# A recurrent attention and two feed-forward layers on one core: the state's decay and part of the values' products moved to ScalarE, with another order of the queues

## The chip, the core and the metric

The kernel runs on one core of one Trainium2 chip. The metric is the device time of one execution in microseconds. TensorE is called PE here, VectorE DVE, ScalarE ACT, GpSimd POOL and SyncE, which issues the transfers, SP.

## The reference

Inputs are r, k, v of 4 sequences, 8 heads, 768 tokens and 48 channels, a decay w and a bonus u for each head and channel, and the weights of two layers. All is float32.

```
for t in range(S):
    cur = einsum('bhd,bhe->bhde', u * k_t, v_t)
    y[t] = einsum('bhd,bhde->bhe', r_t, state + cur)
    state = w * state + einsum('bhd,bhe->bhde', k_t, v_t)
h = relu(y @ w_in)                       # 384 -> 1024
a = conv over 3 tokens of h, by channel
x = (h * sigmoid(a)) @ w_out             # 1024 -> 384
out = x + relu(norm(x) * g @ w_ch1) @ w_ch2   # 384 -> 1536 -> 384
```

## The kernel before, in words

**Attention by chunks.** The 3072 tokens are cut into 24 chunks of 128 (CHUNKS, six to a sequence). Within a chunk the recurrence is a masked product. Chunk m goes through these steps, each a function of the kernel:

- `scale` (DVE, L710): r and k, channels first, times powers of w made at the start.
- `scores` (PE, L407): 16 products k by r into two PSUM banks. `masked` (DVE, L718) twice: the scores times a triangular mask, into `att`.
- `ruk` (POOL, L879 and L881): r*k*u by token. `dots` (DVE, L751): its sum over each head's channels, 8 numbers per token, in `c8`. `cv` (POOL, L894): v times these dots, the token's own term.
- `kd` (POOL, L888): k by token times a table of powers (`powkt`). `kv` (PE, L421): 16 products of it with v, the chunk's contribution to the state.
- `state` (DVE, L736, or L738 and L743): the old state plus that contribution (L738, twice), and then the whole times w to the 128th (L743). The first chunk of a sequence has one multiplication only (L736).
- `y` (PE, L442 and L447): r by the state, plus scores by v. `x_sum` (DVE, L758) adds the term of `cv`. `xt` (PE, L454): three transposes. `xh` (ACT, L556) and `x_low` (DVE, L765) write the high and the low part of the result into the columns that the layers read.

**Layers by units.** The two layers work on 7 units of 440 columns (UNITS). Each float32 product is split in three float32r products of high and low parts (`split_product`, L393 to L395). `mm1` 0 to 7 and `mm2` 0 to 7 are the first layer, `ffn1` 0 to 11 and `ffn2` 0 to 11 the second; each `mm1` or `ffn1` is 9 products. `relu`, `sig` and `hi` are ACT's work on a tile of the first layer, `conv`, `gated` and `low` are DVE's. `x2_hi`, `x2` and `x2_low` take over the first layer's result; `fhi` and `flow` make the second layer's tiles. `sums`, `total`, `square`, `variance`, `root` and `newton` make the norm.

**Order of work.** Each engine's queue is written out by hand: a list for everything up to the end of unit 0 (PE_FIRST, ACT_FIRST, DVE_FIRST, POOL_FIRST, SP_FIRST), and a list that is repeated for units 1 to 6 (PE_PLAN and so on). `each_unit` (L158) runs them. An entry such as ("y", 2) in a PLAN is the third chunk that belongs to the unit: the chunks of unit 0 are 4 to 6 (0 to 3 come ahead of it), of unit 1 they are 7 to 10, then 11 to 13, 14 to 17, 18 to 20 and 21 to 23; unit 6 has none. Steps in LATER are made for the next chunk, and steps in OF_STATE are left out for the last chunk of a sequence. `root` uses a square root, `sig` a sigmoid, and ACT loads a table (ACT_TABLE_LOAD) at each change between them; `table` (L594) is a one-column sigmoid that brings the load forward.

**The start.** DVE makes the powers of w (L668 to L687, a chain of some 30 small instructions that starts when w has been loaded). PE transposes the table (L548), DVE copies it to `powkt` (L840), and then chunks 0 to 3 run in banks that the layers don't use yet. The first product of the layers is ("mm1", 0) of unit 0, at L393. It needs the low part of the first piece of weights (`w_low`, L704). ("means", j) (L541) are six entries of the second layer's preparation each. SP issues every load, in the order of SP_FIRST.

In PE's lists the small float32 products (`scores`, `kv`, `y`, `xt`) stand between the layers' float32r products; a run of such neighbouring entries is called a stretch below.

## Time and profile before

| | |
|---|---|
| median of 3 runs | 633.79 us (632.58 to 634.89) |
| the profiled execution | 634.28 us |
| its span | 632.0 us |
| PE busy | 614.2 us, 97% of the span |
| DVE, ACT, POOL busy | 425.1, 259.0, 141.6 us |
| granted clock over the span | 1.00 |

The span runs from the first to the last instruction of the profiled execution; the 2.28 us between it and the execution's own time lie around it. Busy times are sums over the instructions of an engine, and a matmul's duration includes the time in which its successor has started, so durations on PE overlap; the distance from start to start is the rate.

### The profile page before, as it was taken

The numbers are of one execution on the slowest core, as the hardware profiler recorded it, in microseconds if no ns is written. First come the engines' busy times: TensorE is split into PE (matmuls) and PEld (weight loads), VectorE is DVE, ScalarE is ACT, GpSimd is POOL, SyncE is SP. The second block draws the span as 40 slices with busy tenths as digits, with TensorE's granted clock in tenths as the row PEclk, the third lists the DMA queues.
The fourth block names the chain that finished last, engine by engine and source line by source line (L and its number), as shares of the span: only waits on it lengthen the run. The fifth ranks groups of instructions, "written<-read, shape, count | busy, mean of one in ns | idle before, by whom it ended". The sixth has DMA issues, their size and how long they took to land.

```text
span 632.0 us, 10918 instructions
## 1 busy us (share of the span) xinstructions
PE 614.2 (97%) x4434; PEld 561.2 (89%) x4434; DVE 425.1 (67%) x689; ACT 259.0 (41%) x466; POOL 141.6 (22%) x139
## 2 busy tenths in 40 slices
PE   2999999999999999999999999999999999999997
PEld 2887989999999899999999999999999999999996
DVE  6899987799546597373885556874639746287343
ACT  0256545365323364332643323732327424265340
POOL 4741053401430302331023212032210211000110
PEclk9999999999999999999999999999999999999999
DMA  8980220212202311111022023120020200010001
GB/s 212 321 289 30 89 82 35 68 44 67 67 1 68 110 30 43 63 30 53 29 68 68 0 67 110 31 74 32 31 79 4 67 1 1 1 43 2 0 1 42
DMA packets 15201, 38.78 MB, mean 61 GB/s; under 512 B 2097, under 2 KB 8113, under 8 KB 15153
## 3 DMA queue, kind: packets, MB, share of 16 engines
q1 hardware_dynamic: 15152, 38.10, 19.1%
q8 instruction: 35, 0.57, 0.4%
q14 instruction: 14, 0.11, 0.1%
HBM read 33.37 MB, written 4.72 MB: 60 GB/s over the span
## 4 chain that ended last, share of the span: by engine, by line
PE 95%; DVE 2%; DMA 1%; POOL 1%; issue 1%; SPq 0%; ACT 0%; DVEq 0%; POOLq 0%
PE acc L393 14%; PE hid L393 14%; PE hid L394 13%; PE acc L395 13%; PE hid L395 13%; PE acc L394 13%; PE att_ps L407 3%; PE att_ps L447 3%; PE att_ps L442 2%; PE att_ps L454 1%; PE att_ps L421 1%; DMA raw_n<-rk_n 1%; PE acc L541 1%; PE hid L407 0%; DVE w_raw L698 0%
## 5 line engine op out<-in xcount | busy, mean ns | idle before, releaser
L393 PE MATMUL acc<-ring_hi,w_hi 128*128 128x440 f32 (+1 forms) x420 | 154.1, 367 | 0.0
L395 PE MATMUL acc<-ring_hi,w_lo 128*128 128x440 f32 (+1 forms) x420 | 151.8, 361 | 0.0
L394 PE MATMUL acc<-ring_lo,w_hi 128*128 128x440 f32 (+1 forms) x420 | 151.4, 360 | 0.0
L620 ACT ACTIVATE ring_hi<-hid 128x440 fp32r<-128x440 f32 (+1 forms) x84 | 45.0, 535 | 131.1 <-PE hid L395 128.7
L824 DVE SCALAR_TENSOR_TENSOR ring_lo<-hid,ring_hi 128x440 fp32r<-128x440 f32 (+1 forms) x84 | 51.0, 608 | 68.5 <-ACT ring_hi L620 67.8
L393 PE MATMUL hid<-x_hi,w_hi 128*128 128x440 f32 (+1 forms) x252 | 92.7, 368 | 0.4 <-DVE ring_lo L824 0.3
L394 PE MATMUL hid<-x_lo,w_hi 128*128 128x440 f32 (+1 forms) x252 | 91.6, 363 | 0.0
L395 PE MATMUL hid<-x_hi,w_lo 128*128 128x440 f32 (+1 forms) x252 | 91.1, 361 | 0.0
L393 PEld LDWEIGHTS acc<-ring_hi,w_hi 128*128 128x128 f32 x420 | 78.8, 188 | 6.0
L395 PEld LDWEIGHTS acc<-ring_hi,w_lo 128*128 128x128 f32 x420 | 78.8, 188 | 5.1
L394 PEld LDWEIGHTS acc<-ring_lo,w_hi 128*128 128x128 f32 x420 | 78.8, 188 | 4.6
L879 POOL TENSOR_TENSOR raw_n<-raw_n 128x384 f32<-128x384 f32 x22 | 27.3, 1240 | 239.9 <-DMA raw_n<-rk_n 239.9
L587 ACT ACTIVATE conv_sb<-hid 128x442 f32<-128x442 f32 (+1 forms) x56 | 30.2, 539 | 80.5 <-PE hid L395 71.2
L393 PE MATMUL hid<-xt_hi,w_hi 128*128 128x442 f32 (+1 forms) x168 | 61.9, 368 | 0.3 <-DVE xt_lo L765 0.3
L395 PE MATMUL hid<-xt_hi,w_lo 128*128 128x442 f32 (+1 forms) x168 | 61.1, 364 | 0.0
L394 PE MATMUL hid<-xt_lo,w_hi 128*128 128x442 f32 (+1 forms) x168 | 60.9, 363 | 0.0
L393 PEld LDWEIGHTS hid<-x_hi,w_hi 128*128 128x128 f32 x252 | 47.3, 188 | 5.0 <-DVE ring_lo L824 0.7
L395 PEld LDWEIGHTS hid<-x_hi,w_lo 128*128 128x128 f32 x252 | 47.3, 188 | 3.1
L394 PEld LDWEIGHTS hid<-x_lo,w_hi 128*128 128x128 f32 x252 | 47.3, 188 | 3.0
L774 DVE SCALAR_TENSOR_TENSOR conv_sb<-conv_sb,cw 128x440 f32<-128x440 f32 (+1 forms) x56 | 38.4, 685 | 7.4 <-ACT conv_sb L556 7.3
L894 POOL TENSOR_TENSOR raw_n<-v_sb,c 128x384 f32<-128x384 f32 x22 | 24.0, 1092 | 78.5 <-DVE c L751 78.5
L787 DVE TENSOR_TENSOR ring_lo<-conv_sb,ring_hi 128x440 fp32r<-128x440 f32 (+1 forms) x56 | 35.8, 646 | 7.9 <-ACT ring_hi L556 7.1
(128 smaller groups left out, 960.3 us busy)
## 6 DMA issues: line engine op xcount, KB each, us to landing
rk<-rk_t SPq DMA_DIRECT2D x22, 448.0 KB, 3.7
raw_n<-rk_n SPq DMA_DIRECT2D x22, 384.0 KB, 3.6
w_raw<-weights SPq DMA_DIRECT2D x10, 768.0 KB, 14.5
v_sb<-v_n SPq DMA_DIRECT2D x22, 192.0 KB, 2.4
out<-x SPq DMA_DIRECT2D x18, 220.0 KB, 2.1
first_rk<-rk_t SPq DMA_DIRECT2D x2, 448.0 KB, 11.2
first_raw_n<-rk_n SPq DMA_DIRECT2D x2, 384.0 KB, 11.4
out<-x SPq DMA_DIRECT2D x3, 218.0 KB, 2.2
```

What stands on the lines that cost most here:

```text
L393: mm(ps, lh, rh, start=start, stop=False)
L394: mm(ps, lh, rl, start=False, stop=False)
L395: return mm(ps, ll, rh, start=False, stop=stop)
L407: last = mm(banks_of(m)[q][:, hp * P:(hp + 1) * P], rk_of(m)[rows, 1, hp, :], rk_of(m)[rows, 0, hp, :], start=True, stop=True)
L447: last = mm(y_ps[t, cols], att_of(m)[:, NP * q + hp, t], v_of(m)[:, cols], start=not c, stop=not c or q == 1)
L587: nc.scalar.activation(h_sb[s][:, 0:n + 2], hid[f % 2][:, 0:n + 2], ACT.Relu).then_inc(act_relu, 1)
L620: nc.scalar.activation(ring_hi[:, tile % RING, 0:n], hid[f % 2][:, 0:n], ACT.Relu).then_inc(act_hi, 1)
L774: stt(a, h[:, 0:n], cw[:, f, 0:1], a, ALU.mult, ALU.add).then_inc(dve_c1, 1)
L787: tt(ring_lo[:, f % RING, 0:n], a_sb[f % ROOM][:, 0:n], f32_of(ring_hi[:, f % RING, 0:n]), ALU.subtract).then_inc(dve_pl, 1)
L824: stt(ring_lo[:, tile % RING, 0:n], hid[f % 2][:, 0:n], 0.0, f32_of(ring_hi[:, tile % RING, 0:n]), ALU.max, ALU.subtract).then_inc(dve_fl, 1)
L879: tt(x[:, 0, :], x[:, 0, :], x[:, 1, :], ALU.mult).then_inc(pool_rk, 1)
L894: tt(heads(raw_n_of(m)[:, 0, :]), heads(v_of(m)[:, :]), c8[:, :].unsqueeze(2).to_broadcast([P, H, D]), ALU.mult).then_inc(pool_cv, 1)
```

## The change

ScalarE gets three new pieces of work. `decay` makes the old state times w to the 128th, four instructions of 96 columns with a scale that is read from `w_pow`, into the buffer that `state` then adds to; `state` loses L743 and L736 becomes a copy. So the contribution of a chunk must carry the factor already: four instructions of 128 columns multiply the table of powers by it before PE transposes it. And for chunks 0 to 3 `cv` runs on ScalarE, eight instructions of 48 columns each, in place of one on POOL. `w_low` of the first piece is made in two halves. All lists are written anew: in PE_PLAN ("y", 0), ("kv", 0) and ("xt", 0), ("scores", 1) are one stretch now, in PE_FIRST the second `scores` comes ahead of the first `kv`, and in SP_FIRST w and the constants come ahead of the first 448 KB.

```diff
 PE_FIRST = [
-    ("scores", 0), ("kv", 0), ("scores", 1), ("y", 0), ("kv", 1), ("scores", 2), ("xt", 0), ("y", 1), ("kv", 2),
-    ("xt", 1), ("scores", 3), ("y", 2), ("y", 3), ("kv", 3), ("xt", 2), ("xt", 3), ("means", 0), ("mm1", 0),
-    ("mm1", 1), ("mm1", 2), ("mm1", 3), ("mm1", 4), ("mm1", 5), ("scores", 4), ("means", 1), ("y", 4), ("kv", 4),
...
+    ("scores", 0), ("scores", 1), ("kv", 0), ("y", 0), ("scores", 2), ("kv", 1), ("xt", 0), ("y", 1), ("xt", 1),
+    ("scores", 3), ("y", 2), ("kv", 2), ("y", 3), ("xt", 2), ("kv", 3), ("xt", 3), ("means", 0), ("mm1", 0),
+    ("mm1", 1), ("mm1", 2), ("mm1", 3), ("mm1", 4), ("mm1", 5), ("scores", 4), ("means", 1), ("y", 4),
+    ("means", 2), ("kv", 4), ("mm1", 6), ("mm2", 0), ("mm1", 7), ("xt", 4), ("scores", 5), ("mm2", 1), ("mm2", 2),
+    ("mm2", 3), ("mm2", 4), ("mm2", 5), ("mm2", 6, 7), ("y", 5), ("ffn1", 0), ("ffn1", 1), ("ffn1", 2),
+    ("ffn2", 0), ("ffn1", 3), ("ffn2", 1), ("ffn1", 4), ("scores", 6), ("xt", 5), ("ffn2", 2), ("ffn2", 3),
...
+    ("ffn2", 6), ("ffn1", 10), ("total", 1), ("ffn2", 7), ("y", 6), ("ffn1", 11), ("ffn2", 8), ("kv", 6),
+    ("xt", 6), ("ffn2", 9), ("ffn2", 10, 11)]
 PE_PLAN = [
-    ("mm1", 0), ("mm1", 1), ("scores", 0), ("mm1", 2), ("mm1", 3), ("mm1", 4), ("mm1", 5), ("mm2", 0), ("mm1", 6),
-    ("y", 0), ("kv", 0), ("mm2", 1), ("mm1", 7), ("mm2", 2), ("xt", 0), ("scores", 1), ("mm2", 3), ("mm2", 4),
+    ("mm1", 0), ("mm1", 1), ("mm1", 2), ("scores", 0), ("mm1", 3), ("mm1", 4), ("mm1", 5), ("mm2", 0), ("kv", 0),
+    ("y", 0), ("scores", 1), ("xt", 0), ("mm1", 6), ("mm1", 7), ("mm2", 1), ("mm2", 2), ("mm2", 3), ("mm2", 4),
     ("mm2", 5), ("mm2", 6, 7), ("kv", 1), ("y", 1), ("scores", 2), ("xt", 1), ("ffn1", 0), ("ffn1", 1),
-    ("ffn1", 2), ("ffn2", 0), ("ffn1", 3), ("ffn1", 4), ("ffn2", 1), ("total", 0), ("ffn2", 2), ("ffn2", 3),
-    ("ffn1", 5), ("ffn1", 6), ("ffn2", 4), ("total", 1), ("ffn1", 7), ("ffn2", 5), ("kv", 2), ("y", 2),
-    ("ffn2", 6), ("ffn1", 8), ("ffn1", 9), ("scores", 3), ("xt", 2), ("ffn1", 10), ("ffn2", 7), ("ffn1", 11),
-    ("y", 3), ("ffn2", 8), ("xt", 3), ("kv", 3), ("ffn2", 9), ("ffn2", 10, 11)]
+    ("ffn1", 2), ("ffn1", 3), ("ffn2", 0), ("ffn2", 1), ("total", 0), ("ffn2", 2), ("ffn1", 4), ("ffn1", 5),
+    ("ffn1", 6), ("ffn2", 3), ("ffn2", 4), ("ffn1", 7), ("total", 1), ("ffn2", 5), ("kv", 2), ("y", 2),
+    ("ffn1", 8), ("ffn2", 6), ("scores", 3), ("xt", 2), ("ffn1", 9), ("ffn2", 7), ("ffn2", 8), ("ffn1", 10),
+    ("y", 3), ("kv", 3), ("ffn1", 11), ("ffn2", 9), ("xt", 3), ("ffn2", 10, 11)]
 ACT_FIRST = [
...
+    ("cv", 0), ("decay", 1), ("cv", 1), ("xh", 0), ("decay", 2), ("xh", 1), ("cv", 2), ("w_hi", 0), ("cv", 3),
+    ("xh", 2), ("xh", 3), ("decay", 3), ("w_hi", 1), ("relu", 0), ("relu", 1), ("relu", 2), ("sig", 0),
+    ("relu", 3), ("table",), ("mean", 0), ("sig", 1), ("hi", 0), ("w_hi", 2), ("hi", 1), ("relu", 4), ("sig", 2),
...
 ACT_PLAN = [
...
+    ("decay", 0), ("relu", 0), ("relu", 1), ("sig", 0), ("relu", 2), ("sig", 1), ("hi", 0), ("relu", 3),
+    ("sig", 2), ("sig", 3), ("hi", 1), ("relu", 4), ("hi", 2), ("relu", 5), ("hi", 3), ("sig", 4), ("relu", 6),
+    ("sig", 5), ("xh", 0), ("hi", 4), ("relu", 7), ("sig", 6), ("hi", 5), ("sig", 7), ("hi", 6), ("hi", 7),
+    ("x2_hi", 0), ("x2_hi", 1), ("decay", 1), ("x2_hi", 2), ("x2", 0), ("xh", 1), ("fhi", 0), ("x2", 1),
+    ("fhi", 1), ("x2", 2), ("fhi", 2), ("decay", 2), ("sum_hi", 0), ("fhi", 3), ("square", 0), ("fhi", 4),
+    ("square", 1), ("square", 2), ("fhi", 5), ("fhi", 6), ("sum_hi", 1), ("fhi", 7), ("xh", 2), ("fhi", 8),
+    ("root",), ("fhi", 9), ("decay", 3), ("fhi", 10), ("fhi", 11), ("xh", 3), ("table",)]
...
 DVE_FIRST = [
-    ("scale", 0), ("powkt",), ("scale", 1), ("dots", 0), ("masked", 0, 0), ("masked", 0, 1), ("state", 0),
-    ("masked", 1, 0), ("masked", 1, 1), ("scale", 2), ("state", 1), ("dots", 1), ("x_sum", 0), ("masked", 2, 0),
-    ("scale", 3), ("dots", 2), ("x_sum", 1), ("x_low", 0), ("state", 2), ("masked", 2, 1), ("x_low", 1),
...
+    ("scale", 0), ("powkt",), ("dots", 0), ("scale", 1), ("scale", 2), ("masked", 0, 0), ("masked", 0, 1),
+    ("masked", 1, 0), ("state", 0), ("dots", 1), ("masked", 1, 1), ("x_sum", 0), ("scale", 3), ("state", 1),
+    ("masked", 2, 0), ("x_sum", 1), ("dots", 2), ("masked", 2, 1), ("x_low", 0), ("masked", 3, 0),
+    ("masked", 3, 1), ("x_low", 1), ("dots", 3), ("state", 2), ("w_low", 0, 0), ("x_sum", 2), ("x_sum", 3),
+    ("x_low", 2), ("w_low", 0, 1), ("x_low", 3), ("state", 3), ("scale", 4), ("w_low", 1), ("conv", 0),
...
 DVE_PLAN = [
...
+    ("conv", 0), ("scale", 0), ("conv", 1), ("gated", 0), ("conv", 2), ("masked", 0, 0), ("low", 0), ("conv", 3),
+    ("gated", 1), ("masked", 0, 1), ("gated", 2), ("state", 0), ("low", 1), ("x_sum", 0), ("gated", 3),
+    ("conv", 4), ("conv", 5), ("low", 2), ("low", 3), ("masked", 1, 0), ("gated", 4), ("conv", 6), ("low", 4),
+    ("gated", 5), ("conv", 7), ("gated", 6), ("low", 5), ("gated", 7), ("low", 6), ("x_low", 0), ("dots", 0),
+    ("low", 7), ("scale", 1), ("masked", 1, 1), ("state", 1), ("x_sum", 1), ("x2_low", 0), ("x2_low", 1),
+    ("x2_low", 2), ("x_low", 1), ("flow", 0), ("masked", 2, 0), ("flow", 1), ("flow", 2), ("sum_low", 0),
...
 POOL_FIRST = [
...
+    ("ruk", 0), ("kd", 0), ("ruk", 1), ("kd", 1), ("ruk", 2), ("kd", 2), ("ruk", 3), ("kd", 3), ("ruk", 4),
...
 POOL_PLAN = [
...
+    ("ruk", 0), ("cv", 0), ("kd", 0), ("sums", 0), ("ruk", 1), ("sums", 1), ("ruk", 2), ("kd", 1), ("pad",),
+    ("kd", 2), ("cv", 1), ("ruk", 3), ("kd", 3), ("cv", 2), ("cv", 3)]
 SP_FIRST = [
...
+    ("small", "w"), ("small", "const"), ("load_t", 0), ("small", "u"), ("load_n", 0), ("load_v", 0),
+    ("small", "g"), ("load_t", 1), ("load_t", 2), ("load_n", 1), ("load_n", 2), ("load_t", 3), ("load_v", 1),
+    ("load_v", 2), ("load_n", 3), ("load_v", 3), ("load_w", "in0"), ("load_w", "c1_0"), ("small", "cw"),
+    ("load_w", "in1"), ("loads", 4), ("load_w", "out0"), ("load_w", "out1"), ("load_w", "c1_1"),
...
 def states_made(m):
 
     return (CH - 1) * (m // CH) + min(m % CH + 1, CH - 1)
+
+
+def decays_made(m):
+
+    return (CH - 2) * (m // CH) + min(m % CH, CH - 2)
 
 
 def build(nc, rk_t, rk_n, v_n, w_t, u_row, weights, conv_w, g_ln, consts, out):
...
+        def valued(eng, m):
+
+            if m < AHEAD:
+                eng.wait_ge(act_cv, m + 1)
+            else:
+                eng.wait_ge(pool_cv, m + 1 - AHEAD)
 
...
             def mm1(u, f):
-                if f % 4 == 0:
-                    piece_whole(u, f"in{f // 4}")
+                if u == 0 and f == 0:
+                    pe.wait_ge(lo_first, 1)
+                elif u == 0 and f == 2:
+                    piece_whole(u, "in0")
+                elif f == 4:
+                    piece_whole(u, "in1")
                 if f == 0:
...
-            pe.wait_ge(dve_pow, POW_STEPS)
+            pe.wait_ge(act_tab, 1)
             pe.wait_ge(ld_c, 16)
             for hp in range(NP):
-                last = nc.tensor.transpose(att_ps[2][:, hp * P:(hp + 1) * P], powk[:, hp, :], ident)
+                last = nc.tensor.transpose(att_ps[2][:, hp * P:(hp + 1) * P], att[:, hp, :], ident)
             last.then_inc(pe_tab, 1)
...
+            def cv(m):
+                act.wait_ge(dve_red, m + 1)
+                loaded(act, m, 2)
+                for h in range(H):
+                    cols = slice(h * D, (h + 1) * D)
+                    last = copy(raw_n_of(m)[:, 0, cols], v_of(m)[:, cols], scale=c8[:, h:h + 1])
+                last.then_inc(act_cv, 1)
+
+            def decay(m):
+
+                if m % CH == 0:
+                    return
+                old, behind = state[m % 2], state[(m + 1) % 2]
+                act.wait_ge(dve_st, states_made(m - 1))
+                act.wait_ge(pe_y, m)
+                for hp in range(NP):
+                    last = copy(behind[0:ROWS, hp, :], old[0:ROWS, hp, :], scale=w_pow[0:ROWS, 7, hp:hp + 1])
+                last.then_inc(act_dec, 1)
+
             act.wait_ge(pool_set, 1)
             table(0)
+            act.wait_ge(dve_pow, POW_STEPS + 1)
+            for hp in range(NP):
+                last = copy(att[:, hp, :], powk[:, hp, :], scale=w_pow[:, 7, hp:hp + 1])
+            last.then_inc(act_tab, 1)
             act.wait_ge(ld_gl, 16)
             for k in range(KT):
                 last = copy(mean_g[:, k, :], part[:, 0:1].to_broadcast([P, P]), scale=gl[:, k:k + 1])
...
-            def w_low(turn):
-
-                cols = piece(TURN[turn])
+            def w_low(turn, half=None):
+
+                parts = [x[:, piece(TURN[turn])].rearrange("p (k f) -> p k f", k=KT) for x in (w_lo, w_raw, w_hi)]
+                if half is not None:
+                    parts = [x[:, :, 256 * half:256 * (half + 1)] for x in parts]
+                lo, raw, high = parts
                 dve.wait_ge(act_w, turn + 1)
-                tt(w_lo[:, cols], w_raw[:, cols], f32_of(w_hi[:, cols]), ALU.subtract).then_inc(lo_w, 1)
+                tt(lo, raw, f32_of(high), ALU.subtract).then_inc(lo_first if half == 0 else lo_w, 1)
 
...
                 dve.wait_ge(pe_kv, states_made(m))
                 if m == 0:
                     dve.wait_ge(pool_set, 1)
-                if m:
+                if c:
+                    dve.wait_ge(act_dec, decays_made(m))
+                elif m:
                     dve.wait_ge(pe_y, m)
-                old, behind = state[m % 2], state[(m + 1) % 2]
-                if c:
-                    dve.wait_ge(dve_st, states_made(m - 1))
+                behind = state[(m + 1) % 2]
                 for q in range(2):
                     rows, cols = slice(64 * q, 64 * q + D), slice(q * D, (q + 1) * D)
                     new = banks_of(m)[3][rows, 0:NP * D].rearrange("p (h e) -> p h e", h=NP)
                     if c == 0:
-                        last = tt(behind[rows, :, cols], new, w128(rows, D), ALU.mult)
+                        last = nc.vector.tensor_copy(behind[rows, :, cols], new)
                     else:
-                        last = tt(behind[rows, :, cols], new, old[rows, :, cols], ALU.add)
-                if c:
-                    last.then_inc(dve_add, 1)
-                    dve.wait_ge(dve_add, 4 * (m // CH) + c)
-                    rows = slice(0, ROWS)
-                    last = tt(behind[rows, :, :], behind[rows, :, :], w128(rows, 2 * D), ALU.mult)
+                        last = tt(behind[rows, :, cols], new, behind[rows, :, cols], ALU.add)
                 last.then_inc(dve_st, 1)
 
             def dots(m):
 
                 dve.wait_ge(pool_ruk, m + 1)
                 if m:
-                    dve.wait_ge(pool_cv, m)
+                    valued(dve, m - 1)
                 nc.vector.tensor_reduce(c8[:, :], raw_n_of(m)[:, 0, :].rearrange("p (h d) -> p h d", h=H),
                                         AX.X, ALU.add).then_inc(dve_red, 1)
 
             def x_sum(m):
```

## Rows read from the trace of the kernel before

**Rows 1.** The page, busy time by engine.
```profile
PE 614.2 (97%) x4434; PEld 561.2 (89%) x4434; DVE 425.1 (67%) x689; ACT 259.0 (41%) x466; POOL 141.6 (22%) x139
```

**Rows 2.** PE's waits: line, releaser, us in total, times, longest.
```profile
PE att_ps L548 <- DVE w_pow L686: 9.7, 1, 9.7
PE acc L421 <- POOL raw_n L888: 1.7, 1, 1.7
...
PE att_ps L407 <- DVE first_rk L710: 0.4, 1, 0.4
...
PE att_ps L454 <- DVE raw_n L758: 0.2, 1, 0.2
```

**Rows 3.** Timeline of PE, start: start us, us, line, shape, count, idle before.
```profile
11.12 2.08 PE L407 MATMUL att_ps<-rk 48*128 48x128 f32 x16 [0.34 <-DVE rk L710]
...
14.95 0.88 PE L421 MATMUL acc<-v_sb,raw_n 128*48 128x48 f32 x16 [1.74 <-POOL raw_n L888]
...
26.93 0.85 PE L421 MATMUL acc<-first_v,first_raw_n 128*48 128x48 f32 x16
...
28.63 1.20 PE L407 MATMUL hid<-first_rk 48*128 48x128 f32 x16
...
37.82 0.44 PE L393 MATMUL hid<-xt_hi,w_hi 128*128 128x442 f32 x1 [0.28 <-DVE xt_lo L765]
```

**Rows 4.** Timeline of DVE, start, same columns.
```profile
5.07 0.24 DVE L668 TENSOR_TENSOR powrk<-powrk,w_pow 128x4 f32<-128x4 f32 x2 [3.10 <-DMA w_pow<-w_t]
...
11.87 1.22 DVE L710 TENSOR_TENSOR rk<-rk,powrk 112x1024 f32<-112x1024 f32 x1 [0.33 <-DMA rk<-rk_t]
13.97 0.55 DVE L751 TENSOR_REDUCE c<-raw_n 128x8 f32<-128x384 f32 x1 [0.88 <-POOL raw_n L881]
```

**Rows 5.** DMA issues of the start: count, KB each, median us to landing.
```profile
w_pow<-w_t SPq DMA_DIRECT2D x2, 0.8 KB, 3.3
```

**Rows 6.** Timeline of POOL, start.
```profile
9.94 1.98 POOL L879 TENSOR_TENSOR raw_n<-raw_n 128x384 f32<-128x384 f32 x1 [8.20 <-DMA raw_n<-rk_n]
...
14.86 0.99 POOL L879 TENSOR_TENSOR raw_n<-raw_n 128x384 f32<-128x384 f32 x1
```

**Rows 7.** Timeline of PE in unit 3, at three stretches of float32 products.
```profile
315.09 0.36 PE L395 MATMUL hid<-xt_hi,w_lo 128*128 128x442 f32 x1
315.38 0.39 PE L442 MATMUL att_ps<-state,rk 112*64 112x96 f32 x4
...
317.48 0.47 PE L393 MATMUL acc<-ring_hi,w_hi 128*128 128x440 f32 x1
317.78 0.37 PE L394 MATMUL acc<-ring_lo,w_hi 128*128 128x440 f32 x1
317.99 0.36 PE L395 MATMUL acc<-ring_hi,w_lo 128*128 128x440 f32 x1
...
322.97 0.49 PE L454 MATMUL att_ps<-const,raw_n 128*128 128x128 f32 x3
...
324.49 0.46 PE L393 MATMUL acc<-ring_hi,w_hi 128*128 128x440 f32 x1
...
333.65 0.56 PE L421 MATMUL att_ps<-v_sb,raw_n 128*48 128x48 f32 x16
...
336.84 0.55 PE L454 MATMUL att_ps<-const,raw_n 128*128 128x128 f32 x3
337.14 0.44 PE L393 MATMUL hid<-x_hi,w_hi 128*128 128x440 f32 x1
```

**Rows 8.** Timeline of DVE at the third of these stretches.
```profile
335.86 0.56 DVE L758 TENSOR_TENSOR raw_n<-att_ps,raw_n 128x384 f32<-128x384 f32 x1 [0.28 <-PE att_ps L447]
```

**Rows 9.** Groups by line and shape, ACT: busy us, mean ns, idle before.
```profile
L594 ACT ACT_TABLE_LOAD x7 | 9.0, 1283 | 0.8 <-PEq L950 0.7
L594 ACT ACTIVATE one<-one 128x1 f32<-128x1 f32 x7 | 1.4, 203 | 0.1
L556 ACT ACTIVATE mean_g<-part,gl 128x128 f32<-128x128 f32 x3 | 1.0, 390 | 13.8 <-DMA gl<-g_ln 13.8
```

More of the change, by code:

```diff
@@ new lines @@
+DVE_PLAN = [
+    ("conv", 0), ("scale", 0), ("conv", 1), ("gated", 0), ("conv", 2), ("masked", 0, 0), ("low", 0), ("conv", 3),
[4 more added lines that the diff above has]
+    ("x2_low", 2), ("x_low", 1), ("flow", 0), ("masked", 2, 0), ("flow", 1), ("flow", 2), ("sum_low", 0),
+    ("off_mean", 0), ("flow", 3), ("off_mean", 1), ("dots", 1), ("flow", 4), ("scale", 2), ("off_mean", 2),
+    ("flow", 5), ("flow", 6), ("masked", 2, 1), ("sum_low", 1), ("variance",), ("state", 2), ("x_sum", 2),
+    ("flow", 7), ("masked", 3, 0), ("dots", 2), ("masked", 3, 1), ("x_low", 2), ("flow", 8), ("flow", 9),
+    ("x_sum", 3), ("newton",), ("dots", 3), ("flow", 10), ("flow", 11), ("scaled", 0), ("x_low", 3), ("result", 0),
+    ("scale", 3), ("scaled", 1), ("result", 1), ("scaled", 2), ("state", 3), ("result", 2)]
@@ L148 @@
+    ("load_w", "c1_2"), ("load_w", "c2_0"), ("loads", 5), ("loads", 6), ("load_w", "c2_1"), ("load_w", "c2_2"),
+    ("loads", 7), ("loads", 8), ("results", 0), ("results", 1), ("results", 2)]
 SP_PLAN = [
@@ L151 @@
 LATER = {"scale": 1, "ruk": 1, "dots": 1, "cv": 1, "kd": 1, "loads": 2}
-OF_STATE = {"kv", "state", "kd"}
+OF_STATE = {"kv", "state", "kd", "decay"}
 OF_UNIT = {"mm1", "mm2", "ffn1", "ffn2", "total", "relu", "sig", "hi", "x2_hi", "x2", "fhi", "sum_hi", "square", "root",
@@ L687, in _ @@
             chain(tt(w_pow[:, 7, :], w_pow[:, 6, :], w_pow[:, 6, :], ALU.mult))
-            w128 = lambda rows, n: w_pow[rows, 7, :].unsqueeze(2).to_broadcast([rows.stop - rows.start, NP, n])
             def centre(j):
```

82 lines of the change are left out of this document (29 added, 53 removed), and 10 rows, old and new, of tables (PE_FIRST, POOL_FIRST).

## The prediction

> **What bounds the kernel now.** I read the busy times first: PE is busy for 614.2 of the 632.0 us [rows 1], so a change can pay only by taking time out of PE's own queue or out of its waits. The waits come next: the two that count are 9.7 us for the powers of w and 1.7 us for the first `kd` on POOL [rows 2], both before 15 us, and the rest are of 0.4 us and less. Then the start: the first scores stand at 11.12, the first `kv` at 14.95, and the first product of the layers at 37.82 [rows 3]. From there PE runs without a break, so what happens on DVE, ACT and POOL later is covered, as long as it stays in time. What ends up in the time is thus (a) when the layers begin, (b) how much PE's own sequence takes behind that, and (c) any wait that the new order puts in.
>
> **The stretches of float32 products (b).** In unit 3 the products of the layers follow each other at 0.2 us: 317.78 to 317.99. The step into a stretch is 0.29 (315.09 to 315.38) and the first step behind one 0.30 (317.48 to 317.78), so a stretch costs some 0.1 us at each end on top of its products [rows 7]; a stretch that begins with transposes shows nothing at its first end. Now y with kv takes 2.10 (315.38 to 317.48) and xt with scores 1.52 (322.97 to 324.49), 3.62 together, while all four in one take 3.49 (333.65 to 337.14) [rows 7]. Joining saves 0.13 and one end, 0.1: 0.24 us. PE_PLAN joins exactly these once for each of the units 1 to 5: 5 x 0.24 = 1.2 us less. The other exchanges (the last kv of unit 1 moves from xt to y; in unit 0 the kv of chunks 4 and 6 leave their y) leave the number of stretches as it is; I take them at nothing, with 0.5 us either way. **-1.2.**
>
> **The start (a).** Step by step.
> - w is issued ahead of the 448 KB of the first r and k. Now it lands 3.3 us after its issue, behind them [rows 5], and DVE waits for it until 5.07 [rows 4]. It can't come later than now; the earliest is about 2.5, just behind its issue. I take 3.5. The powers take 4.6 us (5.07 to 9.7, where PE's wait for them ends [rows 2]), so they end at about 8.1.
> - New behind them: four instructions of 128 columns on ACT. The nearest row is the same form: 390 ns each, three in 1.0 us [rows 9], so 1.3 us for four. The table is at 9.4. From the powers' end to the first scores, over the transposes, it is 1.4 us now (9.7 to 11.12), so they start at 10.8, against 11.12 [rows 3]. If w gains nothing, all this is 1.5 us later, still ahead of what follows.
> - DVE has `dots` 0 ahead of `scale` 1 now, and the second scores ahead of the first kv. So the next thing on PE hangs on raw_n 0, which POOL waits for until 9.94 [rows 6]. As much data lies ahead of it as before, but the bulk of it starts some 1 us later, since w and the constants go first; it lands between 0 and 1 us later, I take 0.5. POOL's two products take 1.98 and about as much now; beside an idle DVE they would be 0.99 each [rows 6], so `ruk` ends near 12.5. `dots` 0.55 and `scale` 1.22 [rows 4] follow: 14.3, without 0.5 it would be 13.8.
> - From the first kv at 14.95 to the end of the second y at 26.93 PE now takes 11.98 us [rows 3], with waits of 0.4 and 0.2 us in it [rows 2]. The new order has the same products from its second scores on, 11.3 us: from 14.3 it ends at 25.6, 1.3 us ahead.
> - Part is given back. Now a kv (0.85) [rows 3] stands between the second y and its xt and covers `x_sum`; the new order has xt 1 right behind y 1, so PE waits for an instruction of 0.56 [rows 8] and its handover, 0.65. And kv 2 moves between y 2 and y 3, so that y 3 must wait for `state` 2, which DVE does behind the masks, `x_low` 1 and `dots` 3: 0 to 1.0 us, I take 0.4. Left: 1.3 - 0.65 - 0.4, about 0.3.
> - `cv` on ACT: eight of 48 columns lie between 203 ns (one column) and 390 (128 columns) each [rows 9], 1.6 to 2.6 us for a chunk with their overlap. The one `dots` behind it can wait for that; ACT is nearly idle until 35 us and hides it. The two halves of `w_low` can bring back no more than the 0.28 us for which PE waits at 37.82 [rows 3]; PE does ("means", 0) behind `xt` 3 and ahead of it in both, so I count nothing.
> **-0.3**, between -1.3 and +1.0.
>
> **ACT, units 1 on (c).** A `decay` is four instructions between the same ends, 0.8 to 1.3 us; 16 of them are under 21 us on an engine that is idle 59% of the time. `state` waits for it, and behind `state` stand `x_sum` and `x2_low` on DVE. Decay 1 starts when the second `x2_hi` is done and has until the kv behind `mm2` ends; DVE sheds L743 in exchange. Nothing.
> By the Trainium skill (ScalarE: Activation LUTs, Rules for kernel authors) a multiplication belongs on VectorE, not on ScalarE. By the row, eight small ones cost up to 2.6 us for one instruction of POOL before; by the rule this change would be a loss wherever ACT is on the path, and no row shows it there.
>
> **The table.** In ACT_FIRST `table` stood last, behind `root`; now it stands before the sigmoids, where the sigmoid table is loaded anyway. So the load of 1283 ns [rows 9] that followed `root` falls between `relu` 1 and `sig` 0 of unit 1. Behind it wait relu 2 and 3, and behind those mm1 4 and 5. I give it 1 us of room, no row measures it: **+0.3**, 0 to 1.3.
>
> **Sum.** -1.2 - 0.3 + 0.3 = -1.2 us: 634.28 becomes 633.1. That execution lies 0.49 above the median of the runs, so I forecast 632.6. A measurement of this kernel can hardly tell less than 0.3% (1.9 us) from no change.
>
> **The rivals.**
> 1. *PE's clock rises earlier.* The granted clock stands at 1.00 throughout, but the same 16 scores take 2.08 us at 11.12 and 1.20 at 28.63 [rows 3]: up to the end of the second y PE works at the lower of its two levels, 1.2 GHz, and from 28.63 at 2.4. Before, it had waits of 1.7, 0.4 and 0.2 us [rows 2]. In the new order there is none from 14.3 to the end of the second y, so the rise may come while y 1 runs or before it: that y, some 3 us, would take half. -1.5: 631.1, faster. Against it: from 14.95 PE had only the two short waits in 12 us and still stayed at the lower level. The Trainium skill (TensorE: Matmul & The Clock Gate, Part 1) has the gate follow how busy the array was, on a beat that doesn't start with the kernel; by that rule it could differ between runs of one kernel.
> 2. *The joined stretch waits (slower).* Place: xt 0 of units 1 to 5. `x_sum` 0 now has only the scores (1.1 us) to hide its 0.56, where it had three entries of the layers; DVE has `low` 1 ahead of it, and at the end of the first layer `x_low` 0 and `dots` 0 ahead of `low` 7, for which the last `mm2` waits. For it: the present stretch of four has just 0.4 us of slack (x_sum ends at 335.86 + 0.56, xt starts at 336.84) [rows 7, 8]. Against: the same pattern runs today without a wait. From 0.24 us a unit it eats the gain, from 0.6 it makes the kernel measurably slower; at 0.7 a unit, 3.5 us: 636.1.
> 3. *The start gains nothing or loses*: raw_n 0 comes 1 us late and both new waits are full: +1.0 in place of -0.3, and the table load bites in full: 634.9, no change.
> 4. *The start gains more*: w at 2.5, raw_n on time and no wait for state 2: -1.3, so 631.6, at the edge of faster.
>
> **Chances.** The forecast 0.37, rival 1 0.23, rival 2 0.17, rival 3 0.15, rival 4 0.08. The range 630.2 to 635.9 holds the forecast with its unknown sizes, rivals 1, 3 and 4 and the milder half of rival 2. Faster by over 0.3%: most of rivals 1 and 4 and the better third of the forecast's spread, 0.38; within 0.3%: 0.44; slower: most of rival 2, 0.18.
>
> **What would show it.** Right: the layers start at about 37.5; stretches of about 3.5 us in units 1 to 5, twice in each, with steps of 0.3 behind them; PE's waits behind 38 us under 1 us; a table load before L607 in unit 1. Rival 1 shows in scores 3 or y 1 at half their time. Rival 2 shows as waits of L454 on DVE's raw_n, or of the last mm2 on ring_lo. Wrong altogether: PE's list behind 38 us shrinks by more than 2 us, or waits that sum to more than 1 us.

## The result, and the profile after

The kernel after takes 628.57 us, median of 6 runs (627.73 to 630.49); the kernel before takes 633.88, median of 6 beside them (632.58 to 634.89). The ratio is 0.992 [0.9901, 0.9938]: faster by 0.8%, with its whole interval beyond the 0.3% that count. The forecast was 632.6 in a range from 630.2 to 635.9. The profiled execution took 628.03 us, with a span of 626.3, 5.7 less than before.

The page of the kernel after, busy time by engine, answers to [rows 1]; below it PE's waits, all of them, which answer to [rows 2].

```profile
PE 609.4 (97%) x4434; PEld 558.7 (89%) x4434; DVE 413.7 (66%) x674; ACT 283.8 (45%) x566; POOL 132.6 (21%) x135
```

```profile
PE att_ps L569 <- ACT att L577: 9.1, 1, 9.1
PE hid L424 <- DVE rk L756: 2.0, 1, 2.0
PE acc L459 <- issue: 1.0, 1, 1.0
PE acc L471 <- DVE raw_n L799: 0.7, 1, 0.7
PE att_ps L464 <- issue: 0.2, 1, 0.2
```

ACT has 24.8 us more to do, DVE 11.4 and POOL 9.0 less, and none of it shows among PE's waits: the five stand ahead of 29 us, and there is none in units 0 to 6. The time is in the start again. Timeline of PE there, with the columns of [rows 3]:

```profile
10.15 2.08 PE L424 MATMUL att_ps<-rk 48*128 48x128 f32 x16
14.21 2.08 PE L424 MATMUL hid<-rk 48*128 48x128 f32 x16 [1.98 <-DVE rk L756]
16.22 0.88 PE L438 MATMUL acc<-v_sb,raw_n 128*48 128x48 f32 x16
...
19.15 1.40 PE L424 MATMUL att_ps<-first_rk 48*128 48x128 f32 x16
20.48 0.56 PE L438 MATMUL acc<-v_sb,raw_n 128*48 128x48 f32 x16
...
23.92 0.55 PE L471 MATMUL acc<-const,raw_n 128*128 128x128 f32 x3 [0.66 <-DVE raw_n L799]
24.40 1.16 PE L424 MATMUL hid<-first_rk 48*128 48x128 f32 x16
...
28.68 0.39 PE L459 MATMUL acc<-state,first_rk 112*64 112x96 f32 x4 [0.97 <-issue]
...
33.95 0.76 PE L410 MATMUL hid<-xt_hi,w_hi 128*128 128x442 f32 x1
```

Read the same instruction down the column. The 16 scores take 2.08, 2.08, 1.40 and 1.16 us; before they took 2.08 as late as the third time and 1.20 the fourth, at 28.63 [rows 3]. So PE's clock rises from the lower to the higher of its two levels (1.2 and 2.4 GHz) during the third scores, near 19.7, where before it rose at the beginning of the fourth, near 28.7. From there the small products take 0.55 to 0.65 of what they took. The layers start at 33.95, 3.87 us ahead of 37.82 [rows 3].

DVE and POOL in the same stretch, against [rows 4] and [rows 6]:

```profile
3.00 0.24 DVE L712 TENSOR_TENSOR powrk<-powrk,w_pow 128x4 f32<-128x4 f32 x2 [1.03 <-DMA w_pow<-w_t]
...
12.05 0.55 DVE L792 TENSOR_REDUCE c<-raw_n 128x8 f32<-128x384 f32 x1 [1.24 <-POOL raw_n L922]
12.93 1.23 DVE L756 TENSOR_TENSOR rk<-rk,powrk 112x1024 f32<-112x1024 f32 x1 [0.32 <-DMA rk<-rk_t]
```

```profile
9.95 1.00 POOL L920 TENSOR_TENSOR raw_n<-raw_n 128x384 f32<-128x384 f32 x1 [8.20 <-DMA raw_n<-rk_n]
11.02 1.00 POOL L922 TENSOR_TENSOR raw_n<-raw_n,u_b 128x384 f32<-128x384 f32 x1
```

DVE starts on w 2 us earlier, the first token-major r and k land as late as before (9.95 and 9.94), and POOL's products take 1.00 us each, the first no longer 1.98. And ACT's new work:

```profile
7.78 1.28 ACT L577 ACTIVATE att<-powrk,w_pow 128x128 f32<-128x128 f32 x4 [5.55 <-DVE w_pow L731]
...
12.64 1.91 ACT L577 ACTIVATE raw_n<-v_sb,c 128x48 f32<-128x48 f32 x8 [0.41 <-DVE c L792]
19.32 1.17 ACT L577 ACTIVATE state<-state,w_pow 112x96 f32<-112x96 f32 x4 [4.77 <-PE att_ps L464]
```

Behind the start, a joined stretch of unit 3 in the kernel after, timeline of PE:

```profile
308.46 0.36 PE L412 MATMUL acc<-ring_hi,w_lo 128*128 128x440 f32 x1
308.76 0.56 PE L438 MATMUL att_ps<-v_sb,raw_n 128*48 128x48 f32 x16
...
311.95 0.55 PE L471 MATMUL att_ps<-const,raw_n 128*128 128x128 f32 x3
312.25 0.45 PE L410 MATMUL hid<-xt_hi,w_hi 128*128 128x442 f32 x1
```

308.76 to 312.25 is 3.49 us, the value of the one stretch of four in [rows 7], and now it stands twice in the unit. From the start of the first layer product to the start of the last it is 589.72 us before (37.82 to 627.54) and 588.08 after (33.95 to 622.03), 1.64 less. The stretches give about 1.0 of it (36 in place of 41), the layers' own steps the other 0.65: before, three steps of 0.60, 0.66 and 0.45 us stood in unit 0 (at 57.29, 86.17 and 104.96) where 0.2 is normal, and none does after, while the very first step takes 0.60 in place of 0.27. With 3.87 from the start and some 0.2 behind the last product that makes the 5.7.

### The profile page after: what moved, and what is told of

It reads as the page before. It is cut to its first block, busy times and chain, and to the rows that moved or that the text cites. A ratio compares the mean times of both kernels' runs of the same rounds, so it can differ in the third digit from the quotient of the medians.

```text
span 626.3 us, 11016 instructions
## 1 busy us (share of the span) xinstructions
PE 609.4 (97%) x4434; PEld 558.7 (89%) x4434; DVE 413.7 (66%) x674; ACT 283.8 (45%) x566; POOL 132.6 (21%) x135
## 4 chain that ended last, share of the span: by engine, by line
PE 97%; DMA 1%; DVE 1%; SPq 1%; issue 0%; ACT 0%
PE hid L410 14%; PE hid L411 13%; PE acc L410 13%; PE acc L412 13%; PE hid L412 13%; PE acc L411 13%; PE att_ps L424 4%; PE att_ps L464 3%; PE att_ps L459 2%; PE att_ps L471 2%; DMA rk<-rk_t 1%; PE acc L562 1%; PE att_ps L438 1%; PE hid L424 1%; PE att_ps L550 0%; PE att_ps L551 0%
## 5 line engine op out<-in xcount | busy, mean ns | idle before, releaser
L410 PE MATMUL acc<-ring_hi,w_hi 128*128 128x440 f32 (+1 forms) x420 | 152.3, 363 | 0.0
L815 DVE SCALAR_TENSOR_TENSOR conv_sb<-conv_sb,cw 128x440 f32<-128x440 f32 (+1 forms) x56 | 38.9, 695 | 9.2 <-ACT conv_sb L577 9.0
L628 ACT ACTIVATE conv_sb<-conv_sb 128x440 f32<-128x440 f32 (+1 forms) x56 | 31.5, 564 | 17.2 <-DVE conv_sb L817 17.1
L817 DVE SCALAR_TENSOR_TENSOR conv_sb<-conv_sb,cw 128x440 f32<-128x440 f32 (+1 forms) x56 | 37.9, 677 | 2.0
```

Source lines behind the costliest of these rows:

```text
L410: mm(ps, lh, rh, start=start, stop=False)
L628: nc.scalar.activation(a, a, ACT.Sigmoid).then_inc(act_sig, 1)
L815: stt(a, h[:, 0:n], cw[:, f, 0:1], a, ALU.mult, ALU.add).then_inc(dve_c1, 1)
L817: stt(a, h[:, 2:2 + n], cw[:, f, 2:3], a, ALU.mult, ALU.add).then_inc(dve_cv, 1)
```

## The experiments

The kernels of a group share the runs of the kernel before: 634.19 us for the first four, 633.55, 634.37 and 633.93 for the later groups, 19 to 23 runs each. "Layers start" is the first layer product in the trace (before 37.82, after 33.95).

### The joined stretches and the start, each alone

*e1_plans*: the kernel before with the repeated lists of after, without their decays; the lists up to unit 0 stay.

```diff
 PE_PLAN = [
-    ("mm1", 6), ("y", 0), ("kv", 0), ("mm2", 1), ("mm1", 7), ("mm2", 2), ("xt", 0), ("scores", 1),
+    ("kv", 0), ("y", 0), ("scores", 1), ("xt", 0), ("mm1", 6), ("mm1", 7), ("mm2", 1), ("mm2", 2),
```

> The kernel before with the new lists for units 1 to 6 (no decay in them), and its own start. Theory A (the joined stretches give 0.24 us for each of five units, nothing else does behind the start): 1.2 us faster than before, 0.998, first product of the layers at 37.8 as before. Theory B (most of the 5.3 us comes from the units, by work that ACT took over): no gain here, since nothing was taken over. Theory C (the gain is all at the start): no gain.

632.12 us, 0.997 [0.9958, 0.9981]. From the first layer product to the last it is 588.30 us, 1.42 less than before. So term (b) was right in kind and size: 1.2 forecast, 1.42 in the trace of this kernel. Another 0.5 us is none of the edit's: the layers start at 37.32 in place of 37.82, although the start is that of the kernel before. Its second transposes (`xt` 1) begin 0.28 us earlier, and the clock rises in them and not in the scores behind:

```profile
27.52 0.71 PE L455 MATMUL acc<-const,raw_n 128*128 128x128 f32 x3
28.15 1.16 PE L408 MATMUL hid<-first_rk 48*128 48x128 f32 x16
```

In the kernel before the same two take 0.90 and 1.20. So one and the same start can differ by half a microsecond between two traced executions, with the clock rising at different places.

*e2_start*: the kernel after with the repeated lists of before, and their decays put in; the reverse of the edit above.

> The kernel after with the old lists for units 1 to 6 (decay put in where the new list has it) and the new start and unit 0. Theory A: it keeps the start's 3.9 us and loses 1.2 us: 3.9 to 4.2 us faster than before, 0.9935, first product of the layers at 34. Theory C: as fast as the kernel after. Theory B: no better than before.

629.95 us, 0.9941 [0.9928, 0.9954], layers start 34.42. The start alone brings 3.4 us there, and behind it nothing is gained (589.72 us again). The two parts add up within the noise: 0.30% and 0.59%, against 0.8% together.

### Which part of the start

*e3_loads*: the kernel before with the new order of the loads alone.

```diff
 SP_FIRST = [
-    ("load_t", 0), ("small", "w"), ("small", "const"), ("small", "u"), ("load_n", 0), ("load_t", 1), ("load_n", 1),
+    ("small", "w"), ("small", "const"), ("load_t", 0), ("small", "u"), ("load_n", 0), ("load_v", 0),
```

> The kernel before with the new order of the loads alone. If the start is bound by w's landing, DVE's powers start at 3.0 and the transposes at 7.7, but the second scores still stand behind the first kv, which waits for POOL: PE's idle time before 15 us stays, and the first product of the layers stays within 0.5 us of 37.8. If the loads alone make the clock rise earlier, the second scores or the third take clearly less than 2.08 us, and the start gains 2 us or more.

634.95 us, 1.0014 [1.0005, 1.0023], layers start 38.50. Its first scores start 2 us earlier (9.08), and nothing comes of it: PE's waits for POOL's `kd` grow from 1.7 to 4.3 us, in two pieces, and the layers start 0.7 us later than before.

*e4_old_loads*: the kernel after with the old order of the loads, the reverse edit.

> The kernel after with the old order of the loads. The new step on ACT then comes behind powers that end at 9.8: transposes at 11.1 instead of 9.1. Queue theory: the second scores wait for dots 0 either way and start at 14.2 to 14.5, so the first product of the layers moves by less than 0.5 us, to 34.5 at most. Clock theory: if the second stretch of work stays unbroken from 14.2, the clock rises near 19.4 again; if the rise depends on more than that, it comes later and the start loses up to 3 us.

634.41 us (631.44 to 637.14), 1.0003 [0.9985, 1.002], layers start 38.40. The whole gain is gone. PE's timeline:

```profile
14.79 2.08 PE L424 MATMUL hid<-rk 48*128 48x128 f32 x16 [0.86 <-DVE rk L756]
...
20.92 2.08 PE L424 MATMUL att_ps<-first_rk 48*128 48x128 f32 x16
...
28.85 1.16 PE L424 MATMUL hid<-first_rk 48*128 48x128 f32 x16
...
38.40 0.76 PE L410 MATMUL hid<-xt_hi,w_hi 128*128 128x442 f32 x1
```

Its second scores are only 0.6 us behind those of after; but the third take 2.08, and a wait of 1.4 us stands ahead of the first y. So 0.6 us at 14 has become 4.45 at 38, of which 1.2 are waits and 2.7 the same products' longer durations; the queue theory allowed less than 0.5. Another 1.4 us is lost at 101.8 (a step of 1.60 in place of 0.2), at a product that waits for `ring_lo`: in the old order one piece of weights (768 KB) is issued behind the loads of chunk 7, and ACT, whose queue is in order, stands 4.3 us in front of its `w_hi`:

```profile
100.80 1.49 ACT L577 ACTIVATE w_hi<-w_raw 128x1536 fp32r<-128x1536 f32 x1 [4.29 <-DMA w_raw<-weights]
```

*e8_orders_only*: the kernel before with all lists of after, without the ScalarE work: `cv` 0 to 3 stay on POOL, put into its list between the others, the decay stays on DVE, and the first `w_low` is whole. *e12_work_only*: the kernel after with all lists of before, `cv` and `decay` put into ACT's; the cut below is one line of it, against the kernel before.

```diff
 ACT_FIRST = [
-    ("xh", 0), ("xh", 1), ("w_hi", 0), ("xh", 2), ("xh", 3), ("w_hi", 1), ("mean", 0), ("relu", 0), ("relu", 1),
+    ("cv", 0), ("decay", 1), ("cv", 1), ("xh", 0), ("decay", 2), ("cv", 2), ("xh", 1), ("w_hi", 0), ("cv", 3), ("xh", 2), ("xh", 3), ("decay", 3), ("w_hi", 1), ("mean", 0), ("relu", 0), ("relu", 1),
...
```

> The kernel before with all lists of the kernel after, but no work on ScalarE: the decay stays on DVE, cv of chunks 0 to 3 on POOL, w_low whole. Theory that the order and the loads carry the gain: at least 4 of the 5.3 us, first product of the layers at 34 to 35, stretches joined. Theory that ScalarE's part carries it: a loss of it shows as waits of PE on DVE's state or raw_n, and less than half of the gain stays.

> The kernel after with all lists of the kernel before, decay put into ACT's lists ahead of the state that needs it and cv of chunks 0 to 3 moved to ACT's first list: ScalarE's part without the new order. Theory that this part gives nothing where PE is bound: no gain behind the start, stretches and their cost as before (79 us), and the start 0 to 1.5 us later than before, since the new step on ACT stands ahead of the transposes: 633.5 to 635. Theory that it carries the gain: at least 2 us faster than before.

Without the ScalarE work 631.61 us, 0.9959 [0.9943, 0.9975], layers start 36.89; with that work alone 634.43, 1.0002 [0.9993, 1.001], 38.17. Behind the start the kernel with the orders alone agrees with after: 588.08 us in both. So ScalarE's work pays nothing in the units and nothing by itself; beside the new orders it is worth 2.9 us at the start, together with the halves of `w_low`. The expectation that the orders keep at least 4 of the 5.3 us failed: they keep about half. PE's waits in the kernel with the orders alone:

```profile
PE hid L410 <- DVE rk L713: 3.2, 1, 3.2
PE acc L445 <- issue: 1.6, 1, 1.6
PE acc L457 <- DVE raw_n L761: 0.7, 1, 0.7
```

The second scores start at 14.30, as in after, but the first ones, which have no step on ACT ahead of them, start at 9.06 in place of 10.15. So the pause between them is 3.2 us and not 2.0, and the clock rises near 23.8, inside the second y.

### Is it the clock

In the next kernels PE multiplies constants (float32, 440 columns) into an unused bank; the result does not depend on them.

```diff
+            pe.wait_ge(pool_warm, 1)
+            for i in range(5):
+                mm(acc[2][:, 0:WIDTH], row_sum[:, 0:P], row_sum[:, :], start=True, stop=True)
```

*e5_old_loads_warm* is e4_old_loads with six of them ahead of everything, *e6_before_warm* the kernel before and *e7_after_warm* the kernel after with five.

> The kernel of e4 (after, with the old order of the loads) and, ahead of everything on PE, six products of 128 x 440 in float32 on a constant tile, from about 2.3 us on, into a bank that nothing reads. Clock theory (e4 lost its gain because PE stayed at 1.2 GHz until about 28 us instead of 19): the clock rises before 10 us, the 16 scores at 11.9 take 1.2 us instead of 2.1, and the first product of the layers comes at 34 to 35 instead of 38.4; the time is 4 us below e4, about 630. Load theory (the data of chunks 0 to 3 come later in that order, and the queues wait for them): the scores get faster, but the first product of the layers stays within 1 us of 38.4.

> The kernel before with five such products ahead. Clock theory: most of what the change gained at the start is had by this alone: first product of the layers at 34 to 35 instead of 37.8, time 3 us below before. Queue theory (the new order and ScalarE's part made the start shorter): the queues of DVE and POOL still hold it, less than 1 us is gained.

> The kernel after with five such products ahead. If the clock is all that is left to gain at the start: the products from 14.2 to 19.4 run at 2.4 GHz too, 2 us off 5.2, of which DVE's masks and POOL let through about 1: first product of the layers at 33, time 1 us below after, 627.5. If the second scores' wait (until 14.2) and DVE bind: nothing gained.

634.29 us, 1.0026 [1.0005, 1.0046]; 633.85, 1.0 [0.9988, 1.0012]; 630.42, 0.9941 [0.9922, 0.9961]. None gained, against the clock theory of each expectation, and after became slower (layers start 36.01; 0.9 of its 2.1 us is there at the second scores already, since the first token-major r and k land at 10.92 in that trace, 1.0 us later than in after). The clock did rise: the first scores take 1.16 us in all three. But it fell again. Timeline of PE in e5_old_loads_warm, and its granted clock by stretches (stretch, its length, PE busy, clock, share of the DMA engines, GB/s):

```profile
11.53 1.16 PE L425 MATMUL att_ps<-rk 48*128 48x128 f32 x16
14.85 2.08 PE L425 MATMUL hid<-rk 48*128 48x128 f32 x16 [2.17 <-DVE rk L760]
```

```profile
10.00:15.00 5.00, 1.89 (x22) 0.99 1.06 240
15.00:20.00 5.00, 3.59 (x48) 0.50 1.05 269
20.00:25.00 5.00, 5.00 (x60) 0.50 1.02 391
25.00:30.00 5.00, 4.34 (x57) 0.50 1.03 280
30.00:35.00 5.00, 5.00 (x78) 0.50 1.04 389
```

A wait of 2.2 us, and for the next 20 us PE works at half its clock although it is busy for 90% of them. In e6_before_warm it fell at a wait of 2.6 us (0.50 from 15 to 25, and scores at 1.16 again only at 28.55), in e7_after_warm at one of 4.2 us. The traced execution of e5_old_loads_warm is its slowest, 638.66 us against a median of 634.29, so it shows the fall at its longest. The other executions have no trace, but each has its mean granted clock, and the times of the twelve follow it: 632.47 us at 0.992, 633.92 and 634.09 at 0.991, 634.10 to 634.35 at 0.989, 635.33 at 0.988, 635.81 at 0.986, and 638.41 to 638.66 at 0.984 and 0.983. From the first to the last that is 6 us, and 0.9% of the time is 5.7 us. So the clock costs what it withholds, how long it stays down differs between executions of one kernel, and in these three kernels a clock raised ahead of a pause was worth nothing; the test had to fill the pause.

*e10_old_loads_fill*: e4_old_loads with one constant product between the first kv and the first y, where PE waited 1.4 us anyway. *e13_after_fill*: the kernel after with one between its first two scores. *e11_warm_fill*: the kernel after with five ahead and five between the first two scores.

```diff
-    ("scores", 0), ("scores", 1), ("kv", 0), ("y", 0), ("scores", 2), ("kv", 1), ("xt", 0), ("y", 1), ("xt", 1),
+    ("scores", 0), ("fill", 5), ("scores", 1), ("kv", 0), ("y", 0), ("scores", 2), ("kv", 1), ("xt", 0), ("y", 1), ("xt", 1),
```

> The kernel of e4 (after with the old order of the loads) with one product of 128 x 440 in float32 on a constant tile between the first kv and the first y, where PE waited 1.4 us for the masks. It does no useful work. Theory that unbroken work of PE from the second scores on makes the clock rise early: it rises near 20 instead of 28, the first product of the layers comes at 35 to 36 instead of 38.4, and the time falls by 2 to 3 us against e4 for 1.5 us of work added. Theory that the data's arrival holds e4 back: it stays at 38.4 or gets later.

> The kernel after with a single constant product between the first and the second scores, in the wait of 1.9 us that is left there (1.5 us long at 1.2 GHz, so it delays nothing). If unbroken work raises the clock: PE then works from 9.1 on with pauses under 0.5 us, the clock rises 3 us or more before 19.4, second scores or first kv come out at half their time, first product of the layers near 33.5, 0.5 us below after. If not: third scores at 1.4 us again and nothing gained.

> The kernel after with five constant products ahead, as in e7, and five more between the first and the second scores, where e7 waited 4.2 us and the clock fell again. If the clock falls only because PE waits there: no more lower level at all behind 10 us, second scores, first kv and first y at half their time, first product of the layers at 32 to 33, time 1 us below after, 627.5. If it falls or stays for another cause: the granted clock shows 0.50 between 15 and 20 us again, and nothing is gained.

The one product in the old order of loads brings 2.6 us: layers start at 35.80 in place of 38.40, and 632.33 us, 0.9972 [0.996, 0.9984]. The kernels differ in nothing else but the memset of the constants (0.5 us on POOL). The ratio of e4_old_loads is 1.0003 [0.9985, 1.002], so the two intervals just don't meet. The third scores start at 21.09, 0.2 later than without the product, and take 1.16:

```profile
16.88 0.88 PE L443 MATMUL acc<-v_sb,raw_n 128*48 128x48 f32 x16
...
21.09 1.16 PE L429 MATMUL att_ps<-first_rk 48*128 48x128 f32 x16
22.18 0.56 PE L443 MATMUL acc<-v_sb,raw_n 128*48 128x48 f32 x16
```

From the third scores to the layers it is 14.71 us in place of 17.48, and the two waits on the way are the same in both (0.66 and 0.97). So useless work in a pause makes the kernel 2 us faster, and the durations show how: by the clock. In the kernel after there is little left for it: one product gives 627.81 us, 0.9906 [0.9886, 0.9925], layers start 33.58; ten give 627.37, 0.9891 [0.9877, 0.9904], 33.12, with the clock at 1.00 and every scores at 1.16:

```profile
14.66 1.16 PE L429 MATMUL hid<-rk 48*128 48x128 f32 x16
...
17.57 1.16 PE L429 MATMUL att_ps<-first_rk 48*128 48x128 f32 x16
...
33.12 0.76 PE L411 MATMUL hid<-xt_hi,w_hi 128*128 128x442 f32 x1
```

That is the shortest time here, about 1 us under the kernel after, though the interval overlaps that of e9_after_again beside it (0.9906 [0.9891, 0.9921]). By the traces the lower clock still costs after 0.8 us (33.95 to 33.12).

*e14_before_warm_fill*: the kernel before with five ahead and four between its first scores and first kv. *e15_orders_warm_fill*: e8_orders_only with the ten products of e11_warm_fill. They ask what the queues are worth at a raised clock.

> The kernel before with five constant products ahead and four more between the first scores and the first kv, so that PE's clock is up throughout (if e11's way works here as well). What is left is the old queues: clock theory (the change's start gained by the clock alone) has the first product of the layers at 34 to 34.5 and 3 us below before; if the new order also shortens the queues by themselves, it stands 1 us or more behind e11's 33.1.

> The kernel of e8 (new lists, no work on ScalarE) with the same ten constant products as e11. e11 differs from it only by ScalarE's part (and the halves of w_low). If ScalarE's part counts at the start, by the 0.7 us longer wait for the state that e8 showed and by POOL's cv, the first product of the layers comes 1 us or more behind e11's 33.1; if e8's distance from after was the clock alone (it rose at 24 instead of 19), it stands within 0.5 us of 33.1.

632.65 us, 0.9985 [0.997, 1.0001], layers start 35.87; and 631.85, 0.9968 [0.9954, 0.9982], 35.89. With the same help they come 2.8 us behind e11_warm_fill. In e14_before_warm_fill the clock falls inside the second y at 22.9, behind waits of 1.3 and 1.2 us (0.79 for 20 to 25). In e15_orders_warm_fill all four scores take 1.16, but behind them, inside the third y at 25.3, it falls and is back only near 28.7. PE's two longest waits behind its second scores, and its clock by stretches of 1 us:

```profile
PE acc L450 <- issue: 1.6, 1, 1.6
PE acc L462 <- DVE raw_n L769: 1.3, 1, 1.3
```

```profile
24.00:25.00 1.00, 1.00 (x16) 1.00 1.05 424
25.00:26.00 1.00, 1.00 (x21) 0.67 1.04 306
26.00:27.00 1.00, 1.00 (x21) 0.50 1.10 224
```

The wait of 1.3 ends at 23.44, so the clock falls 2 us behind it, while PE is busy; the wait of 1.6 ends at 30.26, behind the fall. e11_warm_fill has a wait of 1.4 us at the place of the first, and its clock stays. So these kernels lose both ways, by longer waits and by the clock. The traces don't separate the two: none has either of these orders at an unbroken higher clock, and a faster PE would wait longer. The times say a little: three of the twelve executions of e14_before_warm_fill have a mean granted clock of 0.999 or 1.00 and take 630.97, 631.40 and 632.48, and the one of e15_orders_warm_fill with 0.999 takes 630.77, all 3.4 us or more over e11_warm_fill. Of this the stretches and late steps are 1.6 in the first kernel and none in the second. That suggests that the queues are worth 2 us or more by themselves once the clock is up; no trace shows it, and a mean near 1 can also stand for a late first rise.

*e9_after_again* is the kernel after once more.

> The kernel after once more, unchanged, for its trace. If the moment at which PE's clock rises is fixed by the kernel's own sequence, the third scores (chunk 2) start near 19.2 and take 1.4 us again and the first product of the layers stands at 34.0, within 0.2. If it also depends on something outside the kernel, it differs by some us, and the first product of the layers goes with it.

628.31 us, 0.9906 [0.9891, 0.9921], layers start 33.80, third scores 1.37 at 19.04: the clock rises in the same product, 0.2 us earlier.

## Why the prediction was wrong

**The start (a): this step failed.** It said -0.3, between -1.3 and +1.0, and measured -3.87. Its queue part held: w landed at 3.0 (3.5 taken), ACT's four instructions took 1.28 (1.3), the second scores started at 14.21 (14.3), `x_sum` kept PE waiting for 0.66 (0.65) and the third chunk's state for 0.97 (0.4, at most 1.0). That 14.3 was met so closely is partly luck: the token-major r and k were not 0.5 us late, and instead DVE waited 0.32 us for the channels-first ones. What failed is "the new order has the same products from its second scores on, 11.3 us". From the second scores to the end of the second y it took 9.05 us (14.21 to 23.26). The 11.3 us were the price at the lower clock, and I carried it over to a kernel in which the clock rises at 19.7.

Worked out anew: before, from the first kv to the layers, 14.95 to 37.82, it is 22.87 us, of which four waits are 1.39 (0.41, 0.24, 0.46 ahead of the third y, 0.28). After, from the second scores, it is 19.74, of which the waits are 1.80. The same products take 21.48 and 17.94. So: 0.74 earlier at the first of them, +0.41 for waits, and -3.54 for the products. The clock's part of the last is 3.33: scores 2, kv 1, xt 0, y 1, kv 2 and xt 1, the entries that change level, took 8.48 us and take 5.15. Another 0.56 is not the clock: the last product of ("means", 0) counts with its full duration where a wait stands behind it (2.74 for the six) and up to the next start where none does (2.18); 0.33 of that comes back in the first step of the layers, 0.60 for 0.27. The other entries give back 0.35.

One reading in the prediction was short as well: [rows 2] leaves out 0.5 us ahead of the third y, so the waits below the two large ones were not all of 0.4 and less; it changes nothing in the sum.

**Rival 1 was the mechanism**, and it was mis-sized and ranked too low. I priced it as half of one y, 1.5 us. Its sign came true in the form written down ("scores 3 or y 1 at half their time": y 1 takes 1.8 us, 21.45 to 23.26, where it took 3.0), but scores 2, kv 1, xt 0, kv 2 and xt 1 get shorter too. And the argument against it didn't hold: that PE had only two short waits from 14.95 on "and still stayed at the lower level". That doesn't say what the new order does, and why the two differ is not shown: the old one worked from 14.95 to 20.35 without a wait and stayed down, the new one rose 5.5 us after 14.21, with one wait of 0.17. The lengths of the pauses alone don't order the kernels: the pause ahead of 14.95 is 1.7 us, the one ahead of 14.21 is 2.0, and e4_old_loads pauses for 0.9 and for 1.4 us, with its clock up only at the end of the second y, near 27.5. What the runs do show is that filling a pause with work moves the rise by several us, and that a raised clock was gone behind a pause of 2.2 us (e5_old_loads_warm).

By the Trainium skill (TensorE: Matmul & The Clock Gate, Part 1) the gate follows how busy the array has been, on a beat that doesn't start with the kernel; that the rise depends on work and on pauses agrees with these runs. That beat should make the place vary between runs of one kernel, and it does, by some tenths of a microsecond up to 0.8 where there are two traces of one start: in after and its repeat it lies in the same third scores (1.40 at 19.15, 1.37 at 19.04), in e2_start just ahead of them (1.16 at 19.45), and in e1_plans in the transposes ahead of the product in which it rose before. In e4_old_loads the times of ten runs spread over 5.7 us, which may be that, though only one of them has a trace. Of the kernel before, 52 of the 88 executions beside the experiments have a mean granted clock of 1.00 and 12 have 0.993, so in some it had risen and fallen again. The single traces of the kernels here are to be read with that in mind.

**The joined stretches (b)** measured -1.42 alone. In the kernel after it is -1.64, with two things that I took at nothing within 0.5: the last kv of unit 1 in the stretch of y (0.33 less) and the kv of chunk 6 with its xt (0.3 more) cancel, and the late steps in unit 0 are gone, which the prediction had not looked at.

**ACT in units 1 on (c)** was right: a decay takes 1.17 us (0.8 to 1.3) and no product waits for one. `cv` takes 1.91 (1.6 to 2.6). That it is hidden was right too; that it is neutral was not (e8_orders_only, 2.9 us). Without it the second scores come as early, but PE waits 1.65 us in place of 0.97 for the third chunk's state and 0.29 for an `x_sum` behind the whole `w_low`, and the clock rises 4 us later. The Trainium skill's rule against multiplications on ScalarE (ScalarE: Activation LUTs, Rules for kernel authors) would make this a loss where ACT is on the path; here the trace has it off the path (the table, for which PE waits until 9.11, delays the first scores by 1.1 us and not the second), and e12_work_only, with ScalarE's work and nothing else, is at 1.0002.

**The table load**: forecast +0.3. It is where I put it, and nothing waits:

```profile
128.70 1.28 ACT L628 ACT_TABLE_LOAD   x1
129.99 0.57 ACT L628 ACTIVATE conv_sb<-conv_sb 128x440 f32<-128x440 f32 x1
```

PE has no wait there, so the term is 0.

**Rival 2**, the joined stretch that waits, did not come: no wait of L471 or of the last `mm2` in any unit. **Rival 3** had both its waits nearly in full (0.66 and 0.97), but the first r and k were not late. The low end of the range, 630.2, left rival 1 no more than 0.9 us beyond its 1.5; the clock took 3.3.

**What stays open**: why the clock rises at 28.7 before, at 19.7 in after and at 23.8 with the orders alone, where the products are the same and the pause ahead of the second scores is 3.2 us for 2.0; and how much of ScalarE's 2.9 us is the clock. By the sum used above, 0.1 of it is there at the second scores, 1.1 are waits (2.91 for 1.80) and 1.7 the same products at the lower level. How many of these waits the later rise brings with it, no run separates.

## What to carry to other kernels

In the first tens of microseconds ask first at which clock each product runs: take one shape that repeats and read its duration down the timeline, and price a moved product at the level it will have, with both levels as ends of the range. There a pause can cost more than its length and filling it with useless products can pay (2.1 us in e10_old_loads_fill), while products ahead of a pause gained nothing in three kernels. And parts that are each worth nothing alone (the loads' order 1.0014, ScalarE's work 1.0002) can be worth it together, so an experiment on a start takes parts away from the whole as well as adding them to the old kernel.
